# Recurrent attention and two MLPs on one core: decay products on GpSimd, states ahead of inner parts, output stores on two engines

## What is computed

```python
for t in range(S):
    kt, vt, rt, wt = (k[:, :, t], v[:, :, t], r[:, :, t], w[:, :, t])
    cur = np.einsum('bhd,bhe->bhde', u[None] * kt, vt)
    y[:, :, t] = np.einsum('bhd,bhde->bhe', rt, state + cur)
    state = wt[:, :, :, None] * state + np.einsum('bhd,bhe->bhde', kt, vt)
```

## Time and profile before

| | us |
|---|---|
| median of 3 runs | 459.91 (459.24 to 459.96) |
| the profiled execution | 459.98 |
| its span in the trace | 457.9 |
| PE busy | 412.5 (90%) |
| DVE busy | 266.5 (58%) |
| ACT busy | 164.7 (36%) |
| POOL busy | 144.8 (32%) |

### The profile page before, as it was taken

How to read it: one execution, slowest core, us unless ns; L and a number is a source line. 1 busy time by engine, 2 the same in 40 slices (tenths; PEclk the granted TensorE clock), 3 DMA queues, 4 the chain that set the end, 5 groups by cost and what they waited for, 6 DMA issues and landing times.

```text
span 457.9 us, 10469 instructions
## 1 busy us (share of the span) xinstructions
PE 412.5 (90%) x4352; PEld 392.4 (86%) x4352; DVE 266.5 (58%) x541; ACT 164.7 (36%) x334; POOL 144.8 (32%) x151
## 2 busy tenths in 40 slices
PE   1539783997999999999998999999999999999997
PEld 1539772997899889998997999999989999899997
DVE  6998825579853257444547141411489575599562
ACT  3658433434442356521221211211356221356110
POOL 2754400568970056100702056700105201006000
PEclk9977976799999999999999999999999999999999
DMA  8990002666313300000002945300000001000002
GB/s 261 417 362 5 4 3 88 249 178 223 94 63 131 125 7 4 1 1 3 0 1 101 376 117 161 109 1 0 1 0 1 1 1 71 34 1 1 1 8 95
DMA packets 10703, 37.80 MB, mean 83 GB/s; under 512 B 1441, under 2 KB 3233, under 8 KB 9889
## 3 DMA queue, kind: packets, MB, share of 16 engines
q1 hardware_dynamic: 9648, 24.16, 16.5%
q0 software_dynamic: 1008, 12.99, 7.2%
HBM read 34.78 MB, written 2.36 MB: 81 GB/s over the span
## 4 chain that ended last, share of the span: by engine, by line
PE 66%; issue 15%; DVE 10%; POOL 4%; ACT 3%; DMA 1%; SPq 0%; DVEq 0%; POOLq 0%; ACTq 0%
PE PS L1215 18%; PE PS L1217 18%; PE PS L1216 18%; PE PS L1243 4%; DVE WP L865 3%; PE PS L1297 3%; DVE KW L880 2%; PE PS L1308 1%; POOL W1L L505 1%; DVE AT L897 1%; DMA KW<-kw_dram 1%; PE PS L1247 1%; PE PS L1275 1%; PE PS L1395 1%; DVE UN L998 1%
## 5 line engine op out<-in xcount | busy, mean ns | idle before, releaser
L1040 DVE SCALAR_TENSOR_TENSOR HL<-PS,HH 128x384 fp32r<-128x384 f32 x48 | 26.6, 557 | 93.3 <-ACT HH L742 93.3
L742 ACT ACTIVATE HH<-PS 128x384 fp32r<-128x384 f32 x48 | 23.6, 491 | 100.0 <-PE PS L1217 100.0
L1215 PE MATMUL PS<-UTH,W1H 128*128 128x384 f32 x144 | 50.4, 350 | 2.9 <-DVE UTL L1003 2.9
L1215 PE MATMUL PS<-W2H,HH 128*128 128x384 f32 x144 | 50.2, 349 | 0.0
L1217 PE MATMUL PS<-UTH,W1L 128*128 128x384 f32 x144 | 48.7, 338 | 0.0
L1217 PE MATMUL PS<-W2H,HL 128*128 128x384 f32 x144 | 48.6, 338 | 0.0
L1216 PE MATMUL PS<-UTL,W1H 128*128 128x384 f32 x144 | 48.6, 337 | 0.0
L1216 PE MATMUL PS<-W2L,HH 128*128 128x384 f32 x144 | 48.6, 337 | 0.0
L489 POOL TENSOR_TENSOR R<-R,WP 128x384 f32<-128x384 f32 x40 | 39.4, 989 | 23.6 <-ACT RM L654 15.5
L880 DVE TENSOR_TENSOR KW<-KW,WP 128x384 f32<-128x384 f32 x40 | 30.1, 755 | 6.3 <-PE PS L1243 6.0
L1243 PE MATMUL PS<-RM,KW 128*64 128x64 f32 x480 | 20.9, 254 | 13.4 <-DVE KW L880 8.6
(11 more groups left out here) (143 smaller groups left out, 1028.5 us busy)
## 6 DMA issues: line engine op xcount, KB each, us to landing
KW<-kw_dram SPq DMA_DIRECT2D x6, 768.0 KB, 6.2
RAW<-w_dram SPq DMA_DIRECT2D x12, 384.0 KB, 3.3
R<-r_dram SPq DMA_DIRECT2D x8, 384.0 KB, 6.0
V<-v_dram SPq DMA_DIRECT2D x8, 288.0 KB, 6.9
W1H<-w_dram POOLq DMA_DIRECT2D x1, 2304.0 KB, 8.5
W2H<-w_dram POOLq DMA_DIRECT2D x1, 2304.0 KB, 10.2
SGH<-w_sgt_dram POOLq DMA_DIRECT2D x1, 2304.0 KB, 12.6
RAW<-w_sgt_dram SPq DMA_DIRECT2D x6, 384.0 KB, 3.2
```

The lines of the kernel that those rows point to most:

```text
L742: act.activation(HH[:, f % HSLOT, :], hidden_bank(n, f), ACT.Relu).then_inc(s_hh, 1)
L1040: dve.scalar_tensor_tensor(HL[:, f % HSLOT, :], hidden_bank(n, f), 0.0, HH[:, f % HSLOT, :].bitcast(F32), ALU.max, ALU.subtract).then_inc( ...
L1215: pe.matmul(dst, lh, rh, start=start, stop=False)
```

## The change

Four edits, all in the attention of batch 0.

1. DVE keeps only the first product (384 columns) of units 0 and 1 (`first_decays`). The other five of these two units, and all six of units 2 and 3, are made by POOL behind `update_r`, as for units 4 to 7. `wait_decays` counts POOL's semaphore for them.
2. `across(0)` stands in stage 2 ahead of `within(1)`, behind the level 4 scores.
3. In the tail `chunk_states(2)` and `(3)` stand ahead of the inner parts of units 2 and 3.
4. ACT moves the scores of unit 2 between the two stores of units 0 and 1, and the output of unit 3 is stored by DVE (`store_last_y`).

```diff
-            if q < LANES:
-                engine.wait_ge(s_wp_dve, NLEV * q + lev + 1)
+            if q < 2 and lev == 0:
+                engine.wait_ge(s_wp_dve, q + 1)
             else:
-                engine.wait_ge(s_wp_pool, step(q - LANES, lev))
+                engine.wait_ge(s_wp_pool, step(q, lev) - 2)
...
                 update_r(q, lev)
-                if q >= LANES and lev < NLEV - 1:
+                if lev < NLEV - 1:
                     decays(q, lev + 1)
...
             for lev in range(NLEV):
                 for q in range(2):
                     level(q, lev)
+                if lev == 4:
+                    for q in range(2, 4):
+                        decays(q, 0)
...
             store_y(0)
+            move(2)
             store_y(1)
-
-            move(2)
             store_kt(2)
             move(3)
             first_state(2)
             first_state(3)
             prepare(4)
             store_y(2)
-            store_y(3)
...
-            def all_decays(q):
+            def first_decays(q):
 
                 dve.wait_ge(s_kw[q], 16)
-                for lev in range(NLEV):
-                    if lev:
-                        wait_decays(dve, q, lev - 1)
-                    two = decay_of(q, lev).rearrange("p (m two) -> p m two", two=2)
-                    at = wbase(lev + 1)
-                    dve.tensor_tensor(WP[q][:, at:at + (S >> (lev + 1))], two[:, :, 0], two[:, :, 1], ALU.mult
-                                      ).then_inc(s_wp_dve, 1)
+                two = KW[q][:, 1, :].rearrange("p (m two) -> p m two", two=2)
+                at = wbase(1)
+                dve.tensor_tensor(WP[q][:, at:at + S // 2], two[:, :, 0], two[:, :, 1], ALU.mult).then_inc(s_wp_dve, 1)
...
+            def store_last_y():
+
+                col = 3 * PW
+                dve.wait_ge(s_y, 4)
+                rows_x = X[:, 0:NC * D].rearrange("p (c d) -> p c d", d=D)[:, :, col:col + PW]
+                at = y_at(3)
+                dve.tensor_scalar(rows_x.rearrange("p c (a e) -> p a c e", a=2),
+                                  PS[:, at:at + 2, 0:NC * HD].rearrange("p a (c e) -> p a c e", c=NC), 1.0, None, ALU.mult
+                                  ).then_inc(s_x, 1)
...
-            prepare_keys(0)
-            all_decays(0)
-            prepare_keys(1)
-            keep(0, 0)
-            all_decays(1)
-            keep(1, 0)
-            for lev in range(1, NLEV):
+            for q in range(2):
+                prepare_keys(q)
+                first_decays(q)
+            for lev in range(NLEV):
                 for q in range(2):
                     keep(q, lev)
-                if lev in (2, 3):
-                    all_decays(lev)
...
             for k in range(1, NCH - 1):
                 for q in range(2, 4):
                     next_state(q, k)
+            store_last_y()
             token_pairs(2, 4, 0)
...
+                if lev == 4:
+                    across(0)
                 if lev in (3, 4):
                     within(lev - 3, 0)
                     within(lev - 3, 1)
 
-            across(0)
             across(1)
             transpose_k(2)
             transpose_k(3)
+            chunk_states(2)
+            chunk_states(3)
             for q in range(2, 4):
                 within(q, 0)
                 within(q, 1)
-            chunk_states(2)
-            chunk_states(3)
             across(2)
             across(3)
```

## The result

| | before | after |
|---|---|---|
| median | 459.71 us (459.24 to 459.96, 4 runs) | 448.37 us (446.40 to 449.10, 4 runs) |
| profiled execution | 459.98 us, span 457.9 | 449.10 us, span 447.0 |
| mean granted clock there | 0.966 | 0.976 |

The ratio is 0.9748, with an interval of 0.9714 to 0.9781: faster, by 11.3 us of the medians and by 10.9 us of the two profiled executions. The forecast was 446.2 (13.8 less), its range 444.5 to 450.0.

A forecast was written before the change was run, and what follows sets the result against it. Up to 80.6 us, DVE's load in stage 1 and the late-begun state chain in the tail were taken as the bounds, PE behind that. 5.7 + 8.1 = 13.8 off 459.98 gave 446.2 us, range 444.5 to 450.0.

The forecast's parts named there:

- The tail: Scores of level 5 to the end of `across(3)`: state chain and inner parts run side by side, 8.1 us less.
- the walk: Step-by-step timing of the engines through stage 1, stage 2 and the tail, giving 5.7 and 8.1 us.
- the 1.2 us that the prediction names for the two `across`: Tail: `across(2)` and `(3)` at the full clock take 1.60 us instead of 2.78, part of the 8.1.
- Edits 2 and 4 at nothing: Stage 2 and tail: PE is full at `across(0)`, so nothing won; DVE's store, between 0.1 lost and 0.2 gained, taken as 0.
- The first states: End of stage 1: with products on POOL, the first states of units 0 and 1 come 5.7 us earlier.
- the rival on ports: POOL's levels in stages 1 and 2: shared ports make each 3.3 us, not 2.7; time 448.6, chance 0.14.
- The slow rival: Stages 1 and 2: POOL becomes the bound, pairs at 5.0 us, deciding from 4.4; time 466.9, chance 0.03.
- One sign that the prediction named for being wrong: Lower levels of stage 2: the forecast is wrong if POOL idles less than ACT there.
- Stage 2 as a plain shift: First states to the last scores of stage 2: same steps, so the 5.7 us carries through; POOL's 1.5 us lag hidden.
- The shift carried on: Behind `across(3)`: the gain reaches the end one for one; the clock at the transform widens the forecast by 1 us either way.
- The likeliest case of the text: Whole kernel: the forecast as walked, 445.0 to 447.5 us, chance 0.55.
- my two rivals of 448.4 and 448.6: The clock falls in the tail (448.4, chance 0.17); shared ports lengthen POOL's levels in stages 1 and 2 (448.6, chance 0.14).

The follow-up runs named there:

- states_only: Before with only the chunk states of units 2 and 3 moved ahead of their inner parts; 451.66 us, ratio 0.9863.
- tail_only: Before with edits 2 to 4, all decay products still on DVE; 452.40 us, ratio 0.9879.
- across_late: After with `across(0)` put back behind the level 5 scores; 448.42 us, ratio 0.9783.
- store_on_act: After with unit 3's output stored by ACT instead of DVE; 448.11 us, ratio 0.9770.
- tables_later: After with POOL's two table issues behind level 3 of stage 1 instead of level 1; 448.24 us, ratio 0.9791.

## Why the prediction was nearly right, and where it was not

- **The tail.** Predicted 8.1 us less from the end of `across(1)` to that of `across(3)`, measured 8.2 (17.51 to 9.32). Each step of the walk is found: transposes 1.74, chunk states 1.88, four inner phases 3.52, a pause of 0.47 where 0.5 was said, `across(2)` and `(3)` 1.82 with the clock at 1.0. states_only shows that it is edit 3's doing: the state chain, which stood in series with 3.68 us of pause, now lies beside the inner parts. The clock's share is larger than the 1.2 us that the prediction names for the two `across`: the same matmuls went from 5.05 to 3.52 us (inner phases), from 2.82 to 1.88 (chunk states) and from 2.78 to 1.82 (`across`), 3.4 us together by these rows. The other 4.8 are pauses.
- **Edits 2 and 4 at nothing.** Right in the medians: states_only is no slower than tail_only, across_late and store_on_act lie within 0.3 us of after. In the traces edit 2 saves 0.8 us of tail that edit 4's move costs without it, and 0.1 us of the transform's pause is lost to the store on DVE.
- **The first states.** Predicted 5.7 us earlier, measured 4.9. The step that was mis-sized is POOL's work. The walk took 1.28 and 0.55 for an update and a product at level 0, and 2.7 for the two updates and two products of a level. Measured, in POOL's timeline of after:

```profile
13.04 1.01 POOL L489 TENSOR_TENSOR R<-R,WP 128x384 f32<-128x384 f32 x1
14.01 0.66 POOL L474 TENSOR_TENSOR WP<-WP 128x96 f32<-128x96 f32 x1
...
26.96 1.61 POOL L474 TENSOR_TENSOR WP<-KW 128x384 f32<-128x384 f32 x2
...
30.57 1.18 POOL L489 TENSOR_TENSOR R<-R,KW 128x384 f32<-128x384 f32 x1
...
32.50 1.49 POOL L489 TENSOR_TENSOR R<-R,KW 128x384 f32<-128x384 f32 x1
33.96 0.82 POOL L474 TENSOR_TENSOR WP<-WP 128x192 f32<-128x192 f32 x1
```

The pair of units 2 and 3 at level 0 took 4.2 us (30.57 to 34.78, 3.7 by the prediction's numbers), the pairs of level 1 took 3.2 and 3.3, and those of levels 2 and 3 took 2.2 to 2.7. The 2.7 had been read from the level 3 rows of units 4 and 5, and level 3 cost 2.7 in after too. Before's own rows for these units at levels 0 and 1 show more:

```profile
88.02 1.18 POOL L489 TENSOR_TENSOR R<-R,KW 128x384 f32<-128x384 f32 x1
...
90.76 0.50 POOL L474 TENSOR_TENSOR WP<-WP 128x192 f32<-128x192 f32 x1
...
102.36 1.02 POOL L489 TENSOR_TENSOR R<-R,WP 128x384 f32<-128x384 f32 x1
...
104.86 0.46 POOL L474 TENSOR_TENSOR WP<-WP 128x96 f32<-128x96 f32 x1
```

That is 3.2 us for a pair at level 0 and 3.0 at level 1. The walk also has no term for the first products of units 2 and 3, 1.61 us at 26.96. The last update of unit 1 ended at 30.57 where the walk had 29.6, and ACT's copies of unit 3 at 35.18 where it had 33.9; 0.5 of these 1.3 us came back behind them. What is left for the rival on ports is the rest, such as a product of 192 columns at 0.82 in place of 0.50. The Trainium skill, SBUF — State Buffer, section Who interferes with whom, holds that the two engines lock a shared pair of ports; such lengths agree with that, but no run here shows the ports themselves. The slow rival's limit of 4.4 us a pair, of which the prediction said that nothing was near, was nearly met by the one pair of 4.2; and POOL's longest update in before was not 1.41 but 1.53 (at 7.50). One sign that the prediction named for being wrong did come: in the lower levels of stage 2 POOL has no pause, and ACT waits for it.
- **Stage 2 as a plain shift.** This is the step that failed. "From there to the last scores of stage 2 the steps are the same": the steps are, their speed is not. With the clock at 0.50 for some 7 us (43.6 to 50.4), `within(0)` took 1.24 us more, the scores of level 4 0.92 and those of unit 3 at level 3 0.36: 2.52. The pause ahead of `within(0)`, 1.17 in across_late, shrank to 0.82, which leaves 2.17, and the stretch grew from 14.29 to 16.46. I weighed the clock in the tail and at the transform, where before had low stretches, and not in stage 2, where before had none between 40 and 60 us. PE does wait more there once the rest is faster: it was busy for 7.43 us in before's 40 to 50, and for 6.83 in the stretch of after that corresponds, 35.1 to 45.1. That these waits brought the fall is argued, not shown. The fall is not fixed by the kernel's lists: those of across_late and store_on_act are the same up to 44 us, both have the pause of 1.44 us, and the clock fell in one trace and not in the other (17.34 and 14.30). After's own four runs point the same way: 446.40 us at a mean clock of 0.985, and 447.9 to 449.1 at 0.976. By an estimate, 6.8 us at half the clock lower the mean over 447 us by 0.008, about this difference.
- **The shift carried on.** The transform started 10.8 us earlier, the span is 10.9 shorter. Right, and 377.1 to 377.6 us follow that start in all traces but one; the start is again at the lower clock, 69.88 to about 74.3.
- **The sum.** 13.8 less 0.8 (POOL) and 2.2 (clock) is 10.8, of the profiled executions. At the higher clock, 446.40 us in one run, after lies at the forecast of 446.2. The likeliest case of the text was therefore the minority of after's runs, and 448.37 is what my two rivals of 448.4 and 448.6 gave, each for a reason that is not quite the measured one: the clock fell, but in stage 2, and POOL's levels were longer, but by a third of that rival's 2.4 us. That the median lies at these two figures is luck.

What stays open: why a given execution keeps the clock in stage 2. PE of before was busy for 2.73 of the 5 us from 45.00 and kept 1.00, and across_late paused for 1.44 us and kept it too, where store_on_act with the same 1.44 did not. No run holds the clock up in before's tail, so the 3.4 us above are read from rows and not from an experiment; and no trace was taken of before's shortest execution, 455.74 us at a mean clock of 0.985, which is 9.3 above after's 446.40 at the same clock.

## What to carry to other kernels

Where a tail stands still, look for the longest chain of dependent steps and begin it first; here two calls moved by a few lines gave some 8 of 11 us in the profiled executions (5.9 us by their medians), and all else was within 3. A stretch that is taken as shifted needs one more question: how busy is PE in it once what it waits for comes sooner, and at what clock was it before. Work that is moved between DVE and POOL should be priced level by level, from rows of the same size, in which both are as busy as they will be.

## What the runs showed of the hardware

- **Executions of one kernel differed in their granted clock.** Three runs of after were at a mean clock of 0.976 and one at 0.985, 1.5 to 2.7 us apart. A fall in stage 2 cost 1.5 to 3.1 us in five traces, one at 140 us 1.6. With eight filling matmuls, 3.1 us of PE's time, it did not come in stage 2 of the profiled execution, and the median was 1.4 us shorter. A low clock does not always cost: after's trace has 0.82 over 95 to 100 us and 0.84 over 100 to 105, before's has none there, and the time behind the transform's start is the same.
- **A DVE operation on two SBUF operands stood beside several POOL operations in a row**: 6.75 us for one of 0.56, in tables_later. In after the longest was 1.65, and 0.66 the median:

```profile
L877 DVE TENSOR_TENSOR KW<-KW,WP x11: 539/658/1651, 15.4 to 35.8; 128x384 f32<-128x384 f32 x11
```

The row is line 877 of after grouped over 7 to 36 us, with shortest, median and longest in ns. In before the eleven that answer to these (line 880, 7 to 42 us) had 559 and 1179:

```profile
L880 DVE TENSOR_TENSOR KW<-KW,WP x11: 542/559/1179, 18.1 to 41.7; 128x384 f32<-128x384 f32 x11
```

That POOL's unbroken work was the reason is argued from its end (0.42 us ahead), and after's, as unbroken, did not do it; it happened in one profiled execution, and no run took POOL's work away alone.
- **POOL's small products are not cheap in proportion**: in after 0.8 us for 384 columns (two in 1.61), 0.82 or 0.50 for 192, 0.66 or 0.35 for 96.
